# Squaring the clipped ramp on VectorE instead of ScalarE in a two-layer feed-forward kernel

## The chip, the cores and the metric

The kernel runs on one NeuronCore of a Trainium2 chip. The metric is device time in microseconds of one launch; the shorter the better. Weights, queries, keys and values start in device memory and the result ends there.

## What is computed

The reference is a windowed attention with attention sinks, and behind it two dense feed-forward layers of 1536 tokens, model width 512 and hidden width 2048, all in float32. The change touches the nonlinear function of the first feed-forward layer alone:

```python
h = x @ w_in                       # 1536 x 512 times 512 x 2048
beta = 1.0
neg = h <= -beta
pos = h >= beta
g = np.where(pos, h, np.where(neg, 0.0, (h + beta) ** 2 / (4.0 * beta)))
return (g @ w_out)                 # back to 1536 x 512
```

So g is 0 below -1, h above 1, and the square of r = relu(h/2 + 1/2) between. The second layer has an exponential in that place. Attention comes first and its output is the x of the first layer.

## The kernel before

The tokens of the first layer are worked in six chunks of 256 (the code numbers them 0 to 5), those of the second in three chunks of 512. A chunk walks over 16 tiles t of 128 hidden units. TensorE (PE) computes, in this order for each t: `hidden` (12 matmuls into the PSUM bank `h_ps`, lines 495 to 510), `outward` of tile t-2 (12 matmuls into `y_ps`, lines 512 to 527), and then the pieces of attention for the next chunk that the plan `BESIDE` puts on this t: values, transposes, scores. Every weight and activation is split in a high and a low float32r part, and each product takes three matmuls; ScalarE (ACT) casts the high part and VectorE (DVE) subtracts it to get the low one.

A tile of the first layer goes through these steps. ACT computes `ramp` from `h_ps` (line 670) and squares it in place (line 672); DVE takes min and max against h to make `g_full` (line 866, one instruction); ACT casts `g_hi` (`part_hi`, line 662) and DVE subtracts `g_lo` (`part_lo`, line 855). `hidden` of tile t+2 waits until `g_full` of tile t is there (its PSUM bank is then free), and `outward` of tile t waits for `g_lo`. `ramp` and `g_full` each have two buffers.

Each engine runs its own list in order, written out by hand. For one tile DVE's list is: `before_layer` (the split of the next head's keys and queries, lines 784 and 785, and the normalising of the softmax, lines 805 to 811), `part_lo` of the tile before, `activate`, `behind_layer` (row maxima, lines 797 and 800; the split of the sinks, lines 817 and 820) and, in chunk 0 on tiles 0 to 12 and in chunk 5 on even tiles, `split_weights` (line 842; one or two calls). ACT's list runs likewise: split of the head (593, 594), exponentials (603), `part_hi` (662), `activate` (670, 672), copy of the transposed probabilities (608 to 614), `write_x` (619), and the cast half of `split_weights` (644). DVE's line 842 waits for ACT's line 644, and ACT's line 603 waits for DVE's line 800. Heads are worked two per three tiles: scores at tiles 2, 3, 5, 6, 8, 9, 11, 12. GpSimd (POOL) issues the loads of keys, queries and values, and SyncE (SP) those of the weights and the stores. Chunks 0 to 4 carry attention for the chunk behind them; chunk 5 carries none, but splits weights of the second layer.

The constant 0.5 that line 670 uses as its bias lies in a tile `half` of 64 columns, and the row statistics in a tile `small` of 16 columns. Tiles made by `sb0` are for the first layer and are laid out behind `small`; the second layer's tiles reuse their place.

Of the kernel before, what the change touches and what calls it, by code (L numbers as in the profile page):

```python
# [26 lines left out]
ALU = mybir.AluOpType  # L27
ACT = mybir.ActivationFunctionType

P = 128  # L30
# [8 lines left out]
QB = CT // P  # L39
PAIRS = HEADS // 2  # L40
KT = DM // P
FT = DFF // P
# [36 lines left out]
IN_FLIGHT = 2  # L79


def build(nc, qk_first, v_first, q_t, k_t, v_w, v_s, w_in, w_out, ident_d, out, n_sink, window):
# [8 lines left out]
    with ExitStack() as ctx:  # L91
        def sb(name, shape, dt=F32):
            return ctx.enter_context(nc.sbuf_tensor(name, shape, dt))

        def ps(name):
            return ctx.enter_context(nc.psum_tensor(name, [P, 512], F32))

        def sem(name):
            return ctx.enter_context(nc.semaphore(name))
# [5 lines left out]
        xy = sb("xy", [P, KT, TOK])  # L105
        ident = sb("ident", [P, P])

        small = sb("small", [P, IN_FLIGHT * 4 * QB])
        tops, totals = (small[:, n:n + IN_FLIGHT * 2 * QB].rearrange("p (s h j) -> p s h j", s=IN_FLIGHT, h=2)
                        for n in (0, IN_FLIGHT * 2 * QB))  # L110
        top, total = tops[:, 0, :, :], totals[:, 0, :, :]

        first_layer = ctx.enter_context(ExitStack())

        def sb0(name, shape, dt=F32):
            return first_layer.enter_context(nc.sbuf_tensor(name, shape, dt))
# [1 line left out]
        x_hi, x_lo = sb0("x_hi", [P, KT, CT], F32R), sb0("x_lo", [P, KT, CT], F32R)  # L118
        g_hi, g_lo = sb0("g_hi", [P, GR, CT], F32R), sb0("g_lo", [P, GR, CT], F32R)
        ramp, g_full = sb0("ramp", [P, 2, CT]), sb0("g_full", [P, 2, CT])  # L120
        half = sb0("half", [P, 64])


        qs, ks = sb0("qs", [P, 2, CT]), sb0("ks", [P, 2, QB * SW])
# [21 lines left out]
        t_ps, o_ps = ps("t_ps"), ps("o_ps")  # L146
# [16 lines left out]
        ramp_ready, g_hi_ready, x_hi_ready, y_written, w_hi_ready = sem("ramp_ready"), sem("g_hi_ready"), sem("x_hi_ready"), sem("y_written"), sem("w_hi_ready")  # L163
        bent_ready, qk_hi_ready, qk_lo_ready = sem("bent_ready"), sem("qk_hi_ready"), sem("qk_lo_ready")
# [3 lines left out]
        g_ready, g_lo_ready, x_lo_ready, w_lo_ready = sem("g_ready"), sem("g_lo_ready"), sem("x_lo_ready"), sem("w_lo_ready")  # L168
# [8 lines left out]
        def layer_tiles(layer):  # L177

            if layer == 0:
                return CT, (x_hi, x_lo), (g_hi, g_lo), ramp, g_full  # L180
            return CT1, (x1_hi, x1_lo), (g1_hi, g1_lo), ramp1, g1_full
# [236 lines left out]
        def _(pe):  # L418
# [21 lines left out]
            def first_values(p):  # L440
                pe.wait_ge(first_v_loaded[p], 16)
                pe.wait_ge(first_copied, 2 * (p + 1))
                if p >= IN_FLIGHT:
                    pe.wait_ge(x_lo_ready, p - IN_FLIGHT + 1)
                _, o_bank, _, probs_t = flight[p % IN_FLIGHT]

                for block, queries, keys_t in ((0, slice(0, CT), slice(0, CT)), (1, slice(P, CT), slice(CT, CT + P))):
                    for hh in range(2):
                        dims = slice(HD * hh, HD * (hh + 1))
                        last = pe.matmul(o_bank[dims, queries], first_v[p][:, block * P + HD * hh:block * P + HD * (hh + 1)],  # L450
                                         probs_t[hh][:, keys_t], start=(block == 0), stop=(block == 1), skip_group_check=True)
                last.then_inc(first_attn, 1)
# [42 lines left out]
            def hidden(layer, c, t):  # L495

                pe.wait_ge(w_hi_ready, at[layer * NW + 2 * (t // 2)] + 1)
                pe.wait_ge(w_lo_ready, at[layer * NW + 2 * (t // 2)] + 1)
                if t >= 2:
                    pe.wait_ge(g_ready, c * FT + (t - 1))  # L500
                width, (x_hi, x_lo), _, _, _ = layer_tiles(layer)
                o = h_ps[t % 2][:, 0:width]
                f = slice(t * P, (t + 1) * P)
                for k in range(KT):
                    if t == 0:
                        pe.wait_ge(x_lo_ready, c * KT + (k + 1))
                    pe.matmul(o, win_hi[:, k, f], x_hi[:, k, :], start=(k == 0), stop=False)  # L507
                    pe.matmul(o, win_hi[:, k, f], x_lo[:, k, :], start=False, stop=False)  # L508
                    last = pe.matmul(o, win_lo[:, k, f], x_hi[:, k, :], start=False, stop=(k == KT - 1))  # L509
                last.then_inc(h_ready, 1)  # L510

            def outward(layer, c, t):


                pe.wait_ge(w_lo_ready, at[layer * NW + 2 * (t // 2) + 1] + 1)
                pe.wait_ge(g_lo_ready, c * FT + (t + 1))
                _, _, (g_hi, g_lo), _, _ = layer_tiles(layer)
                for m in range(KT):
                    o = y_of(layer, m)
                    begin = t == 0 and (layer == 1 or m % 2 == 0)  # L520
                    cols = slice(m * P, (m + 1) * P)
                    pe.matmul(o, wout_hi[:, t, cols], g_hi[:, t % GR, :], start=begin, stop=False, skip_group_check=True)  # L522
                    pe.matmul(o, wout_hi[:, t, cols], g_lo[:, t % GR, :], start=False, stop=False, skip_group_check=True)  # L523
                    last = pe.matmul(o, wout_lo[:, t, cols], g_hi[:, t % GR, :], start=False, stop=(t == FT - 1), skip_group_check=True)  # L524
                    if layer == 1 and t == FT - 1 and m < KT - 1:
                        last.then_inc(y_done, 1)
                last.then_inc(y_step, 1)
# [36 lines left out]
        def _(act):  # L564
            def first_exponents(p):
                banks = flight[p % IN_FLIGHT][0]
                act.wait_ge(first_neg_max, p + 1)
                if p >= IN_FLIGHT:
                    act.wait_ge(first_probs_t, 2 * (p - IN_FLIGHT + 1))
                for hh in range(2):  # L570
                    for j in range(QB):
                        nc.scalar.activation(seen_probs(p, hh)[:, SEEN_OF[j]], banks[hh][:, SEEN_OF[j]], ACT.Exp,
                                             bias=tops[:, p % IN_FLIGHT, hh, j:j + 1],
                                             accum_out=totals[:, p % IN_FLIGHT, hh, j:j + 1]).then_inc(first_exp, 1)
# [89 lines left out]
            def activate(layer, c, t):  # L664
                act.wait_ge(h_ready, c * FT + (t + 1))
                width, _, _, ramp, g_full = layer_tiles(layer)
                h = h_ps[t % 2][:, 0:width]
                if layer == 0:

                    nc.scalar.activation(ramp[:, t % 2, :], h, ACT.Relu, bias=half[:, 0:1], scale=0.5).then_inc(ramp_ready, 1)  # L670
                    act.wait_ge(ramp_ready, c * FT + (t + 1))
                    nc.scalar.activation(ramp[:, t % 2, :], ramp[:, t % 2, :], ACT.Square).then_inc(bent_ready, 1)  # L672
                else:

                    nc.scalar.activation(ramp[:, 0, :], h, ACT.Relu, scale=-1.0).then_inc(ramp_ready, 1)  # L675
                    act.wait_ge(ramp_ready, c * FT + (t + 1))
                    nc.scalar.activation(g_full[:, t % 2, :], ramp[:, 0, :], ACT.Exp, scale=-1.0).then_inc(bent_ready, 1)  # L677
# [39 lines left out]
            act.wait_ge(half_set, 1)  # L717
            act.wait_ge(zeros_set, 1)

            nc.scalar.activation(t_ps[:, 0:1], half[:, 0:1], ACT.Exp)  # L720
            first_exponents(0)
            first_exponents(1)
            for p in range(PAIRS):
# [23 lines left out]
        def _(dve):  # L747
# [110 lines left out]
            def activate(layer, c, t):  # L858
                width, _, _, ramp, g_full = layer_tiles(layer)
                h = h_ps[t % 2][:, 0:width]  # L860
                g = g_full[:, t % 2, :]
                if layer == 0:


                    dve.wait_ge(bent_ready, c * FT + (t + 1))
                    nc.vector.scalar_tensor_tensor(g, h, 1.0, ramp[:, t % 2, :], ALU.max, ALU.min).then_inc(g_ready, 1)  # L866
                else:

                    dve.wait_ge(bent_ready, c * FT + (t + 1))
                    nc.vector.scalar_tensor_tensor(g, g, -1.0, h, ALU.add, ALU.max).then_inc(g_ready, 1)  # L870
# [110 lines left out]
```

## Time and profile before

| | us |
|---|---|
| three runs | 642.58, 643.86, 646.44 (median 643.86) |
| the profiled execution | 642.58 |
| its span, first to last instruction | 640.9 |
| PE busy | 620.9 (97% of the span) |
| ACT busy | 388.2 (61%) |
| DVE busy | 339.5 (53%) |
| POOL busy | 74.7 (12%) |

The time of the profiled execution is 1.7 us longer than its span. Busy shares are means over stages that differ much: in the first 80 us DVE and ACT are busy nearly all the time, in the second layer (from about 374 us on) less than half of it. TensorE's granted clock was 0.999 of full speed over the whole span. Matmuls overlap one another, so a PE that is "busy" all the time can still have small holes.

### The profile page before, as it was taken

To read this page: it belongs to the slowest core of one execution; us is meant where nothing else is said; L and a number is where in the kernel's file an instruction comes from. 1 tells how busy PE (TensorE), PEld (TensorE's weight loads), DVE (VectorE), ACT (ScalarE), POOL (GpSimd) and SP (SyncE) were. 2 spreads that over 40 slices of the span, in tenths; PEclk is the share of its full clock that TensorE was granted. 3 is DMA by queue.
4 is the path that set the end of the run, shared out by engine and by line. 5 is a ranking of instruction groups with operands and counts; after the bars stand their busy time and mean duration, and the time that the engine had idled before them with its cause. 6 is when DMAs were issued, how large, how long until landed. Compare 5 with 4: busy or idle time off the path is not lost.

```text
span 640.9 us, 12200 instructions
## 1 busy us (share of the span) xinstructions
PE 620.9 (97%) x4164; PEld 554.8 (87%) x4164; DVE 339.5 (53%) x898; ACT 388.2 (61%) x926; POOL 74.7 (12%) x147
## 2 busy tenths in 40 slices
PE   5799999999999999999999999999999999999997
PEld 3688899999999999999999988888888888888886
DVE  6799948666775677477646663322332222322221
ACT  5888867876876787777767764333443333533333
POOL 5213203221221223123000000000000000000000
PEclk9999999999999999999999999999999999999999
DMA  7764212321321222123045600000100000100001
GB/s 272 236 220 144 68 39 73 98 66 31 98 89 39 64 89 89 33 70 103 0 166 164 197 1 0 1 1 1 66 0 0 0 1 1 65 0 0 0 0 65
DMA packets 15276, 42.49 MB, mean 66 GB/s; under 512 B 2852, under 2 KB 4536, under 8 KB 15248
## 3 DMA queue, kind: packets, MB, share of 16 engines
q0 software_dynamic: 7040, 20.57, 10.6%
q1 hardware_dynamic: 8208, 21.56, 9.8%
q8 instruction: 15, 0.25, 0.2%
q14 instruction: 13, 0.11, 0.1%
HBM read 38.98 MB, written 3.15 MB: 66 GB/s over the span
## 4 chain that ended last, share of the span: by engine, by line
PE 85%; DVE 7%; ACT 5%; issue 2%; DMA 0%; ACTq 0%; SPq 0%; DVEq 0%
PE h_ps L507 13%; PE h_ps L509 13%; PE h_ps L508 12%; PE y_ps L522 9%; PE y_ps L524 9%; PE y_ps L523 9%; PE s_ps L524 3%; PE s_ps L523 3%; PE s_ps L522 3%; PE o_ps L490 3%; PE t_ps L470 2%; DVE wout_lo L842 1%; PE s_ps L461 1%; PE s_ps L460 1%; DVE win_lo L842 1%
## 5 line engine op out<-in xcount | busy, mean ns | idle before, releaser
L507 PE MATMUL h_ps<-x_hi,win_hi 128*128 128x256 f32 (+1 forms) x576 | 184.7, 321 | 0.6 <-DVE g_full L866 0.3
L509 PE MATMUL h_ps<-x_hi,win_lo 128*128 128x256 f32 (+1 forms) x576 | 182.8, 317 | 0.0
L508 PE MATMUL h_ps<-x_lo,win_hi 128*128 128x256 f32 (+1 forms) x576 | 182.4, 317 | 0.0
L522 PE MATMUL y_ps<-g_hi,wout_hi 128*128 128x256 f32 (+1 forms) x480 | 145.5, 303 | 1.8 <-DVE g_lo L855 1.8
L524 PE MATMUL y_ps<-g_hi,wout_lo 128*128 128x256 f32 (+1 forms) x480 | 144.9, 302 | 0.0
L523 PE MATMUL y_ps<-g_lo,wout_hi 128*128 128x256 f32 (+1 forms) x480 | 144.8, 302 | 0.0
L507 PEld LDWEIGHTS h_ps<-x_hi,win_hi 128*128 128x128 f32 x576 | 108.1, 188 | 10.1 <-DVE g_full L866 1.1
L508 PEld LDWEIGHTS h_ps<-x_lo,win_hi 128*128 128x128 f32 x576 | 108.1, 188 | 8.4
L509 PEld LDWEIGHTS h_ps<-x_hi,win_lo 128*128 128x128 f32 x576 | 108.2, 188 | 7.2
L870 DVE SCALAR_TENSOR_TENSOR g_full<-g_full,h_ps 128x512 f32<-128x512 f32 x48 | 33.0, 688 | 151.9 <-ACT g_full L677 151.9
L855 DVE TENSOR_TENSOR g_lo<-g_full,g_hi 128x256 fp32r<-128x256 f32 (+1 forms) x144 | 73.7, 512 | 53.3 <-ACT g_hi L662 52.6
L675 ACT ACTIVATE ramp<-h_ps 128x512 f32<-128x512 f32 x48 | 28.8, 599 | 117.4 <-PE h_ps L509 116.8
L662 ACT CAST g_hi<-g_full 128x256 fp32r<-128x256 f32 (+1 forms) x144 | 68.4, 475 | 49.9 <-DVE g_full L870 34.1
L522 PEld LDWEIGHTS y_ps<-g_hi,wout_hi 128*128 128x128 f32 x480 | 90.1, 188 | 7.3 <-DVE g_lo L855 1.4
L523 PEld LDWEIGHTS y_ps<-g_lo,wout_hi 128*128 128x128 f32 x480 | 90.0, 187 | 4.2
L524 PEld LDWEIGHTS y_ps<-g_hi,wout_lo 128*128 128x128 f32 x480 | 90.2, 188 | 3.6
L866 DVE SCALAR_TENSOR_TENSOR g_full<-h_ps,ramp 128x256 f32<-128x256 f32 x96 | 40.2, 419 | 22.1 <-ACT ramp L672 22.0
L670 ACT ACTIVATE ramp<-h_ps,half 128x256 f32<-128x256 f32 x96 | 45.5, 474 | 6.0 <-PE h_ps L509 5.8
L603 ACT ACTIVATE probs<-s_ps,small 128x260 f32<-128x260 f32 x80 | 37.3, 471 | 19.1 <-DVE small L800 19.0
L377 POOL DMA_DIRECT2D ks<-in_k x40 | 22.1, 553 | 209.6 <-DVE q_parts L785 208.0
L672 ACT ACTIVATE ramp<-ramp 128x256 f32<-128x256 f32 x96 | 40.1, 418 | 3.0
L524 PE MATMUL s_ps<-g_hi,wout_lo 128*128 128x512 f32 x96 | 37.8, 394 | 0.0
(109 smaller groups left out, 814.0 us busy)
## 6 DMA issues: line engine op xcount, KB each, us to landing
ks<-in_k POOLq DMA_DIRECT2D x40, 260.0 KB, 2.9
raw<-in_w_in SPq DMA_DIRECT2D x11, 512.0 KB, 4.3
raw<-in_w_out SPq DMA_DIRECT2D x11, 512.0 KB, 3.9
qs<-in_q POOLq DMA_DIRECT2D x40, 128.0 KB, 2.7
vals<-in_v POOLq DMA_DIRECT2D x20, 192.0 KB, 3.0
out_y<-xy SPq DMA_DIRECT2D x12, 256.0 KB, 2.1
xy<-in_w_in SPq DMA_DIRECT2D x5, 512.0 KB, 5.1
xy<-in_w_out SPq DMA_DIRECT2D x5, 512.0 KB, 4.1
```

What stands on the lines that cost most here:

```text
L507: pe.matmul(o, win_hi[:, k, f], x_hi[:, k, :], start=(k == 0), stop=False)
L508: pe.matmul(o, win_hi[:, k, f], x_lo[:, k, :], start=False, stop=False)
L509: last = pe.matmul(o, win_lo[:, k, f], x_hi[:, k, :], start=False, stop=(k == KT - 1))
L522: pe.matmul(o, wout_hi[:, t, cols], g_hi[:, t % GR, :], start=begin, stop=False, skip_group_check=True)
L523: pe.matmul(o, wout_hi[:, t, cols], g_lo[:, t % GR, :], start=False, stop=False, skip_group_check=True)
L524: last = pe.matmul(o, wout_lo[:, t, cols], g_hi[:, t % GR, :], start=False, stop=(t == FT - 1), skip_group_check=True)
L603: nc.scalar.activation(probs[:, j, hh * SW:(hh + 1) * SW], s_ps[j][:, 0:SW], ACT.Exp, bias=top[:, hh, j:j + 1], accum_out=total[:, hh, j:j ...
L662: nc.scalar.copy(g_hi[:, t % GR, :], g_full[:, t % 2, :]).then_inc(g_hi_ready, 1)
L670: nc.scalar.activation(ramp[:, t % 2, :], h, ACT.Relu, bias=half[:, 0:1], scale=0.5).then_inc(ramp_ready, 1)
L672: nc.scalar.activation(ramp[:, t % 2, :], ramp[:, t % 2, :], ACT.Square).then_inc(bent_ready, 1)
L855: nc.vector.tensor_tensor(g_lo[:, t % GR, :], g_full[:, t % 2, :], g_hi[:, t % GR, :].bitcast(F32), ALU.subtract).then_inc(g_lo_ready, 1)
L866: nc.vector.scalar_tensor_tensor(g, h, 1.0, ramp[:, t % 2, :], ALU.max, ALU.min).then_inc(g_ready, 1)
```

## The change

The square of the ramp is no longer computed by ACT but by DVE, as min(r, 1) * r into `g_full`; the last step is then a plain maximum with h. Both forms give the same function: where r is over 1, r is at most h, so the maximum with h gives h. DVE now waits for `ramp_ready` in place of `bent_ready`, and waits for its own first instruction before the second reads its result. The constant 0.5 moves from its own tile of 64 columns into one column of `small`, which grows from 16 to 32 columns, and the first-layer tiles behind move accordingly: those in front of the old place of `half` 64 bytes up, those behind it 192 bytes down.

```diff
-        small = sb("small", [P, IN_FLIGHT * 4 * QB])
+        small = sb("small", [P, 2 * IN_FLIGHT * 4 * QB])
+        half = small[:, IN_FLIGHT * 4 * QB:IN_FLIGHT * 4 * QB + 1]
-        half = sb0("half", [P, 64])
...
                 if layer == 0:
                     nc.scalar.activation(ramp[:, t % 2, :], h, ACT.Relu, bias=half[:, 0:1], scale=0.5).then_inc(ramp_ready, 1)
-                    act.wait_ge(ramp_ready, c * FT + (t + 1))
-                    nc.scalar.activation(ramp[:, t % 2, :], ramp[:, t % 2, :], ACT.Square).then_inc(bent_ready, 1)
...
-            nc.scalar.activation(t_ps[:, 0:1], half[:, 0:1], ACT.Exp)
+            nc.scalar.activation(t_ps[:, 0:1], half[:, :], ACT.Exp)
...
                 if layer == 0:
+                    r = ramp[:, t % 2, :]
+                    dve.wait_ge(ramp_ready, c * FT + (t + 1))
+                    nc.vector.scalar_tensor_tensor(g, r, 1.0, r, ALU.min, ALU.mult).then_inc(bent_ready, 1)
                     dve.wait_ge(bent_ready, c * FT + (t + 1))
-                    nc.vector.scalar_tensor_tensor(g, h, 1.0, ramp[:, t % 2, :], ALU.max, ALU.min).then_inc(g_ready, 1)
+                    nc.vector.tensor_tensor(g, g, h, ALU.max).then_inc(g_ready, 1)
```

## Rows read from the trace of the kernel before

**Rows 1.** The page's first line: the span, and how many instructions.

```profile
span 640.9 us, 12200 instructions
```

**Rows 2.** The chain that ended last: start us, length us, engine, tile, line.

```profile
25.35 0.48 ACT ramp L670
...
91.12 0.48 ACT ramp L670
...
150.68 0.48 ACT ramp L670
151.18 0.43 ACT ramp L672
151.64 0.44 DVE g_full L866
```

**Rows 3.** Busy us (and count) of each engine in two stretches, then clock and DMA.

```profile
64.00:80.00 16.00, 14.95 (x125) 13.85 (x124) 14.71 (x39) 14.38 (x38) 4.69 (x7) 1.00 0.23 69
160.00:192.00 32.00, 32.00 (x279) 30.96 (x278) 24.01 (x81) 25.70 (x75) 8.21 (x16) 1.00 0.31 94
```

**Rows 4.** Line 866 among the groups: count, busy us, mean ns, idle before it.

```profile
L866 DVE SCALAR_TENSOR_TENSOR g_full<-h_ps,ramp 128x256 f32<-128x256 f32 x96 | 40.2, 419 | 22.1 <-ACT ramp L672 22.0
```

**Rows 5.** Timeline of DVE in chunk 0: start, length, instruction, idle before it.

```profile
26.31 0.42 DVE L866 SCALAR_TENSOR_TENSOR g_full<-h_ps,ramp 128x256 f32<-128x256 f32 x1 [0.19 <-ACT ramp L672]
27.25 1.23 DVE L842 TENSOR_TENSOR wout_lo<-xy,wout_hi 128x1024 fp32r<-128x1024 f32 x1 [0.51 <-ACT wout_hi L644]
...
29.31 1.23 DVE L842 TENSOR_TENSOR win_lo<-xy,win_hi 128x1024 fp32r<-128x1024 f32 x1 [0.17 <-ACT win_hi L644]
...
40.41 1.22 DVE L842 TENSOR_TENSOR wout_lo<-xy,wout_hi 128x1024 fp32r<-128x1024 f32 x1 [0.60 <-ACT wout_hi L644]
...
60.64 0.42 DVE L785 TENSOR_TENSOR q_parts<-qs,q_parts 64x256 fp32r<-64x256 f32 x1
61.09 0.17 DVE L805 TENSOR_SCALAR small<-small 128x2 f32<-128x2 f32 x1
...
62.37 0.41 DVE L866 SCALAR_TENSOR_TENSOR g_full<-h_ps,ramp 128x256 f32<-128x256 f32 x1
62.70 0.42 DVE L797 CUSTOM_DVE_ANT_0 s_ps<-s_ps,mask 128x260 f32<-128x260 f32 x1
...
67.41 1.23 DVE L842 TENSOR_TENSOR wout_lo<-xy,wout_hi 128x1024 fp32r<-128x1024 f32 x1 [0.85 <-ACT wout_hi L644]
```

**Rows 6.** Timeline of ACT in chunk 0, around tile 10.

```profile
65.02 0.49 ACT L670 ACTIVATE ramp<-h_ps,half 128x256 f32<-128x256 f32 x1
...
65.86 0.57 ACT L608 COPY probs_t<-t_ps 128x512 f32<-128x512 f32 x1
66.33 1.05 ACT L644 CAST wout_hi<-xy 128x1024 fp32r<-128x1024 f32 x1
```

**Rows 7.** Timeline of PE: the first matmul of outward(12) in chunk 0.

```profile
80.24 0.36 PE L522 MATMUL y_ps<-g_hi,wout_hi 128*128 128x256 f32 x1 [0.20 <-DVE g_lo L855]
```

**Rows 8.** Timeline of DVE in chunk 2: its idle times within three tiles.

```profile
161.59 0.17 DVE L805 TENSOR_SCALAR small<-small 128x2 f32<-128x2 f32 x1 [0.77 <-ACT probs L603]
...
163.71 0.70 DVE L784 TENSOR_TENSOR k_lo<-ks,k_hi 128x520 fp32r<-128x520 f32 x1 [0.76 <-ACT q_parts L594]
...
166.06 0.44 DVE L797 CUSTOM_DVE_ANT_0 s_ps<-s_ps,mask 128x260 f32<-128x260 f32 x1 [0.42 <-PE s_ps L461]
```

**Rows 9.** Timeline of PE in chunk 2: the first matmul of hidden(6).

```profile
165.94 0.28 PE L507 MATMUL h_ps<-x_hi,win_hi 128*128 128x256 f32 x1
```

**Rows 10.** Timelines of DVE and PE at the end of chunk 5.

```profile
367.93 1.23 DVE L842 TENSOR_TENSOR win_lo<-raw,win_hi 128x1024 fp32r<-128x1024 f32 x1 [0.52 <-ACT win_hi L644]
...
371.43 0.43 DVE L855 TENSOR_TENSOR g_lo<-g_full,g_hi 128x256 fp32r<-128x256 f32 x1 [0.47 <-ACT g_hi L662]
...
370.77 0.36 PE L522 MATMUL y_ps<-g_hi,wout_hi 128*128 128x256 f32 x1 [0.54 <-DVE g_lo L855]
...
372.26 0.28 PE L522 MATMUL y_ps<-g_hi,wout_hi 128*128 128x256 f32 x1
```

## The prediction

> **What bounds the kernel now.** I read the chain that ended last first, then the busy times by stretch, then the timelines of DVE, ACT and PE where the chain leaves PE. The span is 640.9 us [rows 1]. The first ramp of each chunk is on that chain [rows 2]: chunk 0 at 25.35, chunk 1 at 91.12, chunk 2 at 150.68. So chunk 1 takes 59.56 us and chunk 0 takes 65.77, 6.2 us more for the same matmuls. The stretches say why [rows 3]: from 160 to 192 us PE is busy for 32.00 of 32 us, DVE for 24.01 and ACT for 25.70; from 64 to 80 us PE has holes (14.95 of 16), and DVE (14.71) and ACT (14.38) are nearly full, since chunk 0 also splits weights. The kernel is bound by PE, except in chunk 0, where DVE and ACT in turn set the pace up to tile 12, and at single points. The change takes a square from ACT for each of the 96 tiles [rows 4] and gives DVE an instruction more. Its effect must come mainly from chunk 0, where 13 of them lie before the point at which PE takes over for good.
>
> **What one tile costs DVE and gives ACT.** DVE keeps one instruction of the old size (the maximum, with one PSUM input; line 866 takes 419 ns [rows 4]) and gets one more in front of it, whose two inputs are the same SBUF tile. Where nothing holds the next instruction, DVE starts it before the last has ended: 62.37 to 62.70, 0.33 us for a length of 0.41, an overlap of 0.08 [rows 5]. Where the next has to come after the last is complete, the overlap is lost: 60.64 to 61.09, 0.45 us for a length of 0.42 [rows 5]. The new instruction has 256 columns too and its follower waits for its completion, so I take 0.42 + 0.03 = **0.45 us per tile**. Below it the nearest rows are 0.33 (a free follower) and 0.17 + 0.03 = 0.20 (line 805, with hardly any columns). Above it I see nothing dearer for 256 columns except an instruction that pays its length and gap twice, 0.90. I keep 0.20 and 0.90 as ends and sit on 0.45, from the row nearest in size and kind of follower.
>
> The Trainium skill, "VectorE: DVE Perf Modes", section "The DRAIN you can't avoid", says that a semaphore between two VectorE instructions costs nothing extra, since the next waits for the pipe to empty anyway. The rows don't bear that out: 0.33 against 0.45. By that rule the price is the free one, 0.33, and the sum below is +0.7 us instead of +2.0; it is within the third rival.
>
> ACT loses the square. From the ramp to the copy behind the square it now takes 65.02 to 65.86, 0.84 us; without the square it is the ramp's 0.49 less the 0.10 by which a free follower overlaps on ACT (65.86 to 66.33 for a length of 0.57), so 0.39 [rows 6]. ACT gains **0.45 per tile**; bounds: 0.33 and 0.53, the square's length of 0.43 [rows 2] less and plus the overlap.
>
> The way of one tile through both engines keeps its length: ramp at 150.68, square at 151.18, line 866 from 151.64 to 152.08 [rows 2]; new: the ramp ends at 151.16, then 0.03 to the other engine, 0.42, 0.03, 0.42: 152.06. Where PE waits for g_full of tile 0 at a chunk's start, nothing changes.
>
> **Chunk 0, step by step.** The chain here is a loop of three tiles (two heads). DVE splits weights (line 842) and works through two tiles up to the row maxima (line 800); ACT takes over with exponentials, part_hi, ramp, square, a copy and the weight cast, and DVE's next line 842 waits for that cast. The DVE piece holds two of the new instructions, the ACT piece one square. A new line 842 starts at the later of two: ACT's cast, 0.45 earlier against the lag so far, or DVE's own list, 0.45 later less its slack. The slack is the idle time before line 842 plus the overlap of 0.08 that a free follower would have: 0.51 + 0.08 and 0.17 + 0.08 in tiles 0 and 1, 0.60 + 0.08 in tile 4, 0.85 + 0.08 in tile 10 [rows 5] and, alike, in tile 7. As lags against the old times:
> - tile 0: line 866 was 0.19 late for want of the square [rows 5]; 0.45 - 0.19 - 0.59 = -0.33.
> - tile 1: DVE -0.33 + 0.45 - 0.25 = **-0.13**; ACT, 0.45 earlier twice, comes before that.
> - tiles 2 and 3 +0.90; tile 4: DVE +0.77 + 0.45 - 0.68 = **+0.54**, ACT +0.77 - 0.45 = +0.32.
> - tiles 5 and 6 +0.90; tile 7: DVE 1.44 + 0.45 - 0.93 = +0.96, ACT **+0.99**.
> - tiles 8 and 9 +0.90; tile 10: DVE 1.89 - 0.48 = +1.41, ACT **+1.44**.
> - tiles 11 and 12 +0.90: **+2.34**. Then DVE makes g_lo of tile 12, for which PE waits until 80.24 [rows 7].
>
> From there PE works through its list, so the 2.3 us stay. 13 x 0.45 would be 5.9; DVE's idle time takes up more than half. At tile 7 and 10 the two engines come out even: neither has anything left to give.
>
> **Chunks 1 to 4.** DVE's idle times in three tiles are 0.77, 0.76 and 0.42 [rows 8], 1.95 us, and it gets 1.35. Followed through: the maxima of tile 3 come 0.45 later, so do the exponentials and, in front of tile 4, line 805 at 161.59. Tile 4 adds 0.45; ACT, without its square, begins copy and head split on time, so line 784 is 0.90 - (0.76 + 0.08) = 0.06 late. Tile 5 adds 0.45 and line 797 is 0.51 - (0.42 + 0.08) = 0.01 late, where it waits for PE's scores. So the lag is gone once per loop. The latest result in between is g_full of tile 4, 0.90 late; it stands directly before line 784 in DVE's list, so it is there by 163.85, and PE takes it for hidden of tile 6 at 165.94 [rows 9]. Cost 0; what it costs if this cover goes is a rival below.
>
> **Chunk 5 and the rest.** PE waits 0.54 us at 370.77 for g_lo of tile 14 [rows 10]. On DVE that stands behind two weight splits, the first of which (367.93) waits 0.52 for ACT's cast, and the cast stands behind a square. The cast comes 0.45 earlier. DVE must be ready as early: its slack there is 0.52 + 0.08 = 0.60, and where line 866 itself waited for the square, as it does for 22.0 us in sum over the kernel [rows 4], the pair in its place ends no later than it did. So g_lo of tile 14 comes 0.45 earlier. Tile 15 then waits for its own way through both engines, which is no shorter: its g_lo ends at 371.86 and PE starts some 0.1 later, at about 371.96 against 372.26 [rows 10]. PE gains 0.3. The second layer is PE's alone and its instructions are the same. Setting one column in place of 64 lies in the first microsecond, before the loads have landed. The shift of tiles by 64 or 192 bytes I take as 0: no row shows any effect of a tile's place, and the only bound either way is the spread of the three runs, 3.9 us.
>
> **Sum.** 2.3 - 0.3 = +2.0 us: the profiled execution goes from 642.58 to 644.6, its span from 640.9 to 642.9. That execution was the fastest of three and the median lies 1.28 higher, so I predict 645.9.
>
> **Rivals.**
> - *Nothing is absorbed.* If DVE's idle before line 842 isn't filled, because ACT's cast comes no earlier (the copy before it waiting for PE's transposes), each of 13 tiles costs 0.45: 5.85 - 0.3 = +5.6, 649.5. For it: both engines wait for each other in a loop. Against: the copy at 65.86 followed the square at once [rows 6], with nothing else awaited.
> - *Chunks 1 to 4 become DVE's.* With the three overlaps DVE's slack in a loop is 0.85 + 0.84 + 0.50 = 2.19 us [rows 8], so it is the bound from 2.19 / 3 = 0.73 us per tile on. At 0.90, the upper end, each loop loses 3 x 0.17 = 0.51; with 4 loops (8 heads) in each of 4 chunks that is 8 us, and chunk 0 gets 13 x 0.45 = 5.9 more than in the walk: +16, about 660. Against: no instruction of 256 columns costs that.
> - *The new instruction is cheap.* At 0.33 the same walk gives +1.0 in chunk 0, at 0.20 it gives -0.3; in all +0.7 or -0.6, 643.3 to 644.6.
> - *ACT's relief wins.* Five pieces of the chain in chunk 0 hold a square (tiles 0, 1, 4, 7, 10), one in chunk 5. If ACT decides at all of them, it takes off 5 x 0.45 = 2.25, against eight DVE instructions on the chain (tiles 2, 3, 5, 6, 8, 9, 11, 12): faster from a price below 2.25 / 8 = 0.28 on; at a price of 0 it would be -2.6, 641.3. Against: 0.20 is the least that any row shows, and there it is worth half a microsecond.
>
> **How the numbers follow.** The walk as worked out 0.58, nothing absorbed 0.17, chunks 1 to 4 0.07, a cheap instruction 0.12, ACT's relief 0.06. About 0.5% (3.2 us) is what a measurement of this kernel can tell from no change. Slower by more: the second and third case and 0.05 of the first by the spread of runs, 0.29. Faster by more: 0.05 of the last, with the shift of tiles. The rest, 0.66, is within. The range goes from 643.0 (a cheap instruction and a little spread) to 650.0 (nothing absorbed, and half a microsecond).
>
> **What would show it.** Right if in the profile after the first ramps of chunk 0 and 1 are about 68.1 us apart and the later ones still 59.5; if the new instruction is 0.42 us long and 0.45 ahead of the maximum; if DVE's idle before line 842 in chunk 0 is nearly gone; if DVE's busy time is up and ACT's down by 40 us each; if PE's wait at the end of chunk 5 splits into about 0.1 at tile 14 and 0.2 at tile 15. Wrong if chunks 1 to 4 grow, if the pair is spaced otherwise, or if idle time stays before line 842.

## The result and the profile after

| | before | after |
|---|---|---|
| median of six runs, us | 643.87 (642.58 to 646.44) | 651.98 (650.91 to 654.3) |
| ratio, 95% interval | | 1.0127 (1.0104 to 1.0149) |
| profiled execution, us | 642.58 | 650.88 |
| its span, us | 640.9 | 649.1 |

The change made the kernel slower by 1.3%, 8.1 us. The forecast was 645.9 with a range of 643.0 to 650.0; the time lies outside it, and every rival but one (660, for chunks 1 to 4) ended below it too.

The page of after, its span, busy times and chain by engine:

```profile
span 649.1 us, 12200 instructions
...
PE 628.1 (97%) x4164; PEld 558.4 (86%) x4164; DVE 377.9 (58%) x994; ACT 349.4 (54%) x830; POOL 74.7 (12%) x147
```

DVE is busy 38.4 us more and ACT 38.8 us less, as the change intends. But PE is busy 7.2 us more, with the same 4164 instructions. That is the first sign that something acts on PE itself, and not through a wait.

Next I took the first ramps of the chunks, as in [rows 2]. The timeline of ACT in after (start, length, instruction, idle time before it):

```profile
25.23 0.47 ACT L670 ACTIVATE ramp<-h_ps,small 128x256 f32<-128x256 f32 x1 [0.42 <-PE h_ps L509]
...
93.44 0.47 ACT L670 ACTIVATE ramp<-h_ps,small 128x256 f32<-128x256 f32 x1 [0.19 <-PE h_ps L509]
...
153.36 0.47 ACT L670 ACTIVATE ramp<-h_ps,small 128x256 f32<-128x256 f32 x1 [0.19 <-PE h_ps L509]
...
380.89 0.60 ACT L673 ACTIVATE ramp<-h_ps 128x512 f32<-128x512 f32 x1 [1.63 <-PE h_ps L509]
```

From such rows of both traces comes the table on which everything below rests, in us:

| stretch | before | after | difference |
|---|---|---|---|
| start to the first ramp | 25.35 | 25.23 | -0.12 |
| chunk 0 | 65.77 | 68.21 | +2.44 |
| chunks 1 to 4 | 59.56, 59.45, 59.55, 59.21 | 59.92, 59.97, 59.94, 59.75 | +1.81 |
| chunk 5 | 47.74 | 47.87 | +0.13 |
| second layer, from its first ramp on | 264.27 | 268.21 | +3.94 |

Chunk 0 is where the walk put its 2.3 us. Nearly all of the rest, 5.75 us, lies in stretches for which the prediction had 0, and the largest piece lies in the second layer, where no instruction was changed. The first 512-token chunk of that layer, stretch by stretch (start and end, length, then busy us and count of PE, PEld, DVE, ACT, POOL, then clock, DMA share, GB/s), first before:

```profile
376.63:464.52 87.89, 87.89 (x385) 72.12 (x384) 27.94 (x39) 36.57 (x59) 0.00 (x0) 1.00 0.03 13
```

and after:

```profile
380.89:470.13 89.24, 89.24 (x385) 72.35 (x384) 27.96 (x39) 36.48 (x60) 0.00 (x0) 1.00 0.03 12
```

PE is busy all the time in both, the granted clock is 1.00 in both, DVE, ACT and DMA do the same work. So the 384 matmuls have become dearer. The timeline of PE in before, four matmuls in a row:

```profile
400.46 0.39 PE L522 MATMUL s_ps<-g_hi,wout_hi 128*128 128x512 f32 x1
400.69 0.39 PE L523 MATMUL s_ps<-g_lo,wout_hi 128*128 128x512 f32 x1
400.92 0.39 PE L524 MATMUL s_ps<-g_hi,wout_lo 128*128 128x512 f32 x1
401.15 0.39 PE L507 MATMUL h_ps<-x_hi,win_hi 128*128 128x512 f32 x1
```

and the same four in after:

```profile
405.09 0.39 PE L522 MATMUL s_ps<-g_hi,wout_hi 128*128 128x512 f32 x1
405.32 0.40 PE L523 MATMUL s_ps<-g_lo,wout_hi 128*128 128x512 f32 x1
405.55 0.40 PE L524 MATMUL s_ps<-g_hi,wout_lo 128*128 128x512 f32 x1
405.79 0.40 PE L507 MATMUL h_ps<-x_hi,win_hi 128*128 128x512 f32 x1
```

Three starts take 0.69 us before and 0.70 after. A difference of 1.5% can't be read from rows with two decimals; it can from a stretch: 87.89 / 384 = 0.2289 us from start to start before, 89.24 / 384 = 0.2324 after. In the code of this layer nothing differs but where its tiles lie. Hence the theory for the experiments: *place*, the time of a matmul depends on the address of what it reads. Its rival: *computation*, the new instruction on DVE costs more than the walk says, beside PE's work too.

Medians of the same kernel differ by some 2 us from one set of runs to another (before: 643.2, 645.1, 643.8, 644.0), because some of its executions spend 2 to 4 us more in front of the first ramp (27.5 to 29.0 us in such profiles instead of 25.2 to 26.2), so ratios are taken within a set, and lengths of chunks, which this doesn't touch, are compared across all profiles and are the finer measure.

### The profile page after: what moved, and what is told of

Same layout as the page of the kernel before. It is cut to its first block, busy times and chain, and to the rows that moved or that the text cites. A ratio compares the mean times of both kernels' runs of the same rounds, so it can differ in the third digit from the quotient of the medians.

```text
span 649.1 us, 12200 instructions
## 1 busy us (share of the span) xinstructions
PE 628.1 (97%) x4164; PEld 558.4 (86%) x4164; DVE 377.9 (58%) x994; ACT 349.4 (54%) x830; POOL 74.7 (12%) x147
## 4 chain that ended last, share of the span: by engine, by line
PE 86%; DVE 9%; ACT 2%; issue 1%; DMA 0%; ACTq 0%; SPq 0%; DVEq 0%
PE h_ps L507 13%; PE h_ps L509 13%; PE h_ps L508 13%; PE y_ps L522 10%; PE y_ps L523 9%; PE y_ps L524 9%; PE s_ps L522 3%; PE s_ps L523 3%; PE s_ps L524 3%; PE o_ps L490 3%; PE t_ps L470 2%; DVE wout_lo L840 1%; PE s_ps L461 1%; PE s_ps L460 1%; DVE win_lo L840 1%
## 5 line engine op out<-in xcount | busy, mean ns | idle before, releaser
L507 PE MATMUL h_ps<-x_hi,win_hi 128*128 128x256 f32 (+1 forms) x576 | 186.7, 324 | 0.8 <-DVE g_full L866 0.4
L522 PE MATMUL y_ps<-g_hi,wout_hi 128*128 128x256 f32 (+1 forms) x480 | 147.0, 306 | 1.8 <-DVE g_lo L853 1.8
L670 ACT ACTIVATE ramp<-h_ps,small 128x256 f32<-128x256 f32 x96 | 45.5, 474 | 6.0 <-PE h_ps L509 6.0
L864 DVE SCALAR_TENSOR_TENSOR g_full<-ramp 128x256 f32<-128x256 f32 x96 | 40.3, 420 | 9.4 <-ACT ramp L670 9.2
L866 DVE TENSOR_TENSOR g_full<-g_full,h_ps 128x256 f32<-128x256 f32 x96 | 40.4, 421 | 3.3
```

The lines of the kernel that those rows point to most:

```text
L864: nc.vector.scalar_tensor_tensor(g, r, 1.0, r, ALU.min, ALU.mult).then_inc(bent_ready, 1)
L866: nc.vector.tensor_tensor(g, g, h, ALU.max).then_inc(g_ready, 1)
```

## The experiments

For orientation in what follows: the weights (`win_hi`, `win_lo`, `wout_hi`, `wout_lo`) lie in front of `small`, and what a matmul streams past them (`x_hi`, `x_lo`, `g_hi`, `g_lo` and the second layer's `x1_hi`, `g1_hi` and so on) lies behind it. The change moves all of the latter by 64 or -192 bytes, which is the same step of 64 within 256 (that 256 is the period is shown by e5 and e8 below).

**Splitting the change (e1, e2).** e1 is the kernel before with the change's layout alone:

```diff
-        small = sb("small", [P, IN_FLIGHT * 4 * QB])
+        small = sb("small", [P, 2 * IN_FLIGHT * 4 * QB])
+        half = small[:, IN_FLIGHT * 4 * QB:IN_FLIGHT * 4 * QB + 1]
-        half = sb0("half", [P, 64])
```

> The kernel before with only the tiles moved: small has 32 columns, half is one of them, ACT still squares. The measured change is +8.2 us of span, of which chunk 0 shows +2.4 (as the walk of the prediction gave), chunks 1 to 4 about +0.4 each and each chunk of the second layer +1.3, though no instruction differs there. Theory P (the place of the tiles in SBUF slows PE's matmuls, pitch 0.2289 to 0.2324 us in the second layer): this kernel loses about 5.9 us, 649.8, with 16-tile chunks of the second layer at 89.2 us and chunk 0 unchanged at 65.8. Theory D (the work moved to DVE costs it, also later): this kernel is as before, 643.9, second-layer chunks 87.9 us. Theory R (the difference of the second layer is chance of that profiled execution): also 87.9.

e2 is the other half: the square on DVE, with `small` and `half` as before.

```diff
-                    act.wait_ge(ramp_ready, c * FT + (t + 1))
-                    nc.scalar.activation(ramp[:, t % 2, :], ramp[:, t % 2, :], ACT.Square).then_inc(bent_ready, 1)
...
+                    nc.vector.scalar_tensor_tensor(g, r, 1.0, r, ALU.min, ALU.mult).then_inc(bent_ready, 1)
```

> The kernel after with the tiles where they were before: small 16 columns, half a tile of 64 columns; DVE squares and ACT does not. Theory P: +2.0 us against before, 645.9, the number of the prediction: chunk 0 at 68.2 us, chunks 1 to 4 at 59.5, second-layer chunks 87.9. Theory D: +8, 652.0, and second-layer chunks 89.2.

Measured: e1 651.87 us, ratio 1.0113 (1.0085 to 1.0141); e2 645.57 us, 1.0028 (1.0011 to 1.0044). The second layer's first chunk of e1, stretch as above:

```profile
381.89:471.13 89.24, 89.24 (x385) 72.34 (x384) 27.96 (x39) 36.59 (x59) 0.00 (x0) 1.00 0.03 12
```

and of e2 chunk 0, chunk 1 and the same chunk of the second layer:

```profile
25.25:93.34 68.09, 61.74 (x510) 57.28 (x509) 62.04 (x163) 49.85 (x123) 13.46 (x23) 1.00 0.40 126
93.34:152.90 59.56, 59.23 (x510) 56.85 (x509) 47.08 (x148) 38.46 (x111) 13.67 (x25) 1.00 0.23 71
...
377.58:465.47 87.89, 87.89 (x385) 72.11 (x384) 27.95 (x39) 36.51 (x59) 0.00 (x0) 1.00 0.03 11
```

e1 has after's second-layer chunk to the hundredth (89.24) with before's computation, and chunks 1 to 4 of 59.96, 59.98, 59.95, 59.70. Its ratio says 7.3 us, more than the 5.9 expected; its chunks add up to 6.3. e2 has before's (87.89), chunks of 59.56, 59.56, 59.55, 59.33, and a chunk 0 of 68.09. So the two halves of the change act apart: the layout costs 1.8 us in chunks 1 to 4 and 4.0 in the second layer; the computation costs 2.3 in chunk 0. Its rival, that the computation costs more beside PE's work, falls: 0.2 us in chunks 1 to 4 together. e2 has one oddity: its chunk 5 takes 46.24 instead of 47.74, though no tile was moved, and that is why its profiled span is only 0.9 us above before's. That execution is also the shortest of e2's twelve (643.52 against a median of 645.57), so not every execution need have it.

The oddity is not e2's alone: at this distance matmuls of 256 columns keep one of two pitches, 0.1133 or 0.1178 us, and both occur in before. In chunk 2 of before there are 22 steps from 152.34 to 154.83, 0.113 us each, and 22 from 185.82 to 188.41, 0.118 each (timeline of PE, first and last row of each stretch):

```profile
152.34 0.28 PE L508 MATMUL h_ps<-x_lo,win_hi 128*128 128x256 f32 x1
154.83 0.28 PE L524 MATMUL y_ps<-g_hi,wout_lo 128*128 128x256 f32 x1
...
185.82 0.28 PE L508 MATMUL h_ps<-x_lo,win_hi 128*128 128x256 f32 x1
188.41 0.28 PE L524 MATMUL y_ps<-g_hi,wout_lo 128*128 128x256 f32 x1
```

Nearly all the rest of before's chunks 1 to 5 runs at the longer pitch; one more such stretch lies in chunk 4. e2's chunk 5 runs at the shorter one in one piece of 334 steps, from behind the chunk's first tile up to PE's wait at tile 14, and the ten steps behind the wait at tile 15 are back at 0.118. So the pitch is kept while nothing interrupts the stream and can change where something does. What chooses between the two isn't shown.

**Absolute place or distance (e3, e4).** e3 puts a spare tile of 128 bytes behind `small`, so only what is streamed moves; e4 puts one of 64 bytes in front of the weights, so all moves together.

```diff
+        spare = sb("spare", [P, 32])      # e3: behind small
...
+        spare0 = sb("spare0", [P, 16])    # e4: in front of win_hi
```

> The kernel before with a spare tile of 32 columns (128 bytes) behind small, so that all tiles behind it lie 128 bytes up. If what matters is the place of the matmuls' moving tiles within 128 bytes (now 64 past a multiple of 128, after the change on a multiple), this kernel is as fast as before, 643.9, pitch 0.229. If any move away from the old place costs, or the period is longer, it is slower, up to 650.

> The kernel before with a spare tile of 16 columns (64 bytes) in front of the weights, so that weights and all other tiles lie 64 bytes up together. If it is the absolute place of the moving tiles that matters, this kernel is slow like the changed one, near 650 with a pitch of 0.232. If it is their place relative to the weights, it is as before, 643.9 with 0.229.

Measured: e3 643.92, ratio 1.0000 (0.9978 to 1.0022); e4 643.72, 0.9998 (0.9977 to 1.0018). e4 is before again in every chunk (59.56, 59.45, 59.54, 59.22; 87.89). e3's equal total hides two effects of opposite sign, as its chunk 1 and the second layer show:

```profile
94.18:152.65 58.47, 58.16 (x510) 55.81 (x509) 40.69 (x132) 44.65 (x127) 13.66 (x25) 1.00 0.25 72
...
374.24:463.84 89.60, 89.60 (x385) 72.19 (x384) 27.96 (x39) 36.59 (x59) 0.00 (x0) 1.00 0.03 12
```

The attention chunks are 1.1 us shorter each, the second layer's 1.7 longer. It isn't the address of a tile that counts but the distance from the weights to it, and the two widths of matmul (256 and 512 columns) like different distances. For 256 columns the step from before's distance to e3's brings no new pitch but more of the shorter one: e3's chunk 1 has 0.1178 in its tiles 1 to 3 and 0.1135 to 0.114 from tile 4 on, where before has 0.1178 in all of these.

**Mapping the distance (e5, e7, e8, e9).** Here the first layer's tiles and the second layer's move separately, by a spare tile in front of `x_hi` (n columns) and one in front of `g1_hi` (m columns); the second layer's reuse the place of the first, so their shift doesn't include n. e5: n 32, m 128; e7: 48, 48; e8: 64, 64; e9: 32, 48.

```diff
+        spare = sb0("spare", [P, n])
         x_hi, x_lo = sb0("x_hi", [P, KT, CT], F32R), sb0("x_lo", [P, KT, CT], F32R)
...
+        spare1 = sb("spare1", [P, m])
```

> The kernel before with its first-layer tiles 128 bytes up (a spare tile of 32 columns) and its second-layer tiles 512 bytes up (a spare tile of 128 columns), weights untouched. With everything 128 up the chunks with attention took 58.46 us in place of 59.5 and those of the second layer 89.6 in place of 87.9. Theory P (only the distance of moving tile and weights counts, layer by layer, and it repeats with the weights' own step of 512 bytes): 4 x 1.1 + 1.4 less in the first layer, the second unchanged at 87.9, so about 5.7 us less than before: 637.5, faster than both kernels. If it does not repeat after 512 bytes, the second layer stays at 89 or more and the whole at 643. If the two layers' times were tied in some other way (clock, chance), nothing like 637 comes.

> The kernel before with the tiles of both layers 192 bytes up, 256 past the weights' step where it was 64. If a distance that is a multiple of 128 is bad (as 128 was), chunks with attention 59.95 us and second-layer chunks 89.2 or more: 650. If the times fall and rise with a period of 128 bytes only, they are those of 128. If the distance acts over the whole 512 bytes, other numbers than the three known.

> The kernel before with the tiles of both layers 256 bytes up, distance 320. With a period of 256 bytes it is as before: 59.5 and 87.9 us per chunk, 643.2. With a period of 128 bytes likewise. With one of 512, other numbers: it then says which way the second layer goes beyond 192, where it had 89.6.

> The computation of the kernel before, with each layer's tiles where its matmuls were fastest so far: first-layer tiles 128 bytes up (58.4 us per chunk with attention), second-layer tiles 192 bytes up (87.04 us per chunk). Theory P: 4 x 1.1 + 1.3 + 3 x 0.86 = 8.3 us less than before, 635 us. If the two gains don't add, no better than 639.

Measured: e5 639.07, ratio 0.9909 (0.9880 to 0.9939); e7 645.98, 1.0011 (0.9990 to 1.0032); e8 643.51, 0.9989 (0.9968 to 1.0009); e9 636.61, 0.9884 (0.9853 to 0.9915). Chunk 1 and the second layer's first chunk of e7:

```profile
93.97:154.13 60.16, 59.92 (x510) 57.54 (x509) 40.82 (x132) 44.83 (x127) 13.62 (x25) 1.00 0.24 70
...
382.79:469.83 87.04, 87.04 (x385) 72.07 (x384) 27.90 (x39) 36.56 (x59) 0.00 (x0) 1.00 0.03 12
```

and the second layer's first chunk of e9:

```profile
373.14:460.18 87.04, 87.04 (x385) 72.07 (x384) 27.91 (x39) 36.56 (x59) 0.00 (x0) 1.00 0.03 12
```

Shifts of 256 (e8) and 512 bytes (e5's second layer, 87.90) give before's chunks back. With the distance of before counted as 64, chunks 1 to 3 and the second layer of all these profiles fit one table (chunk 5 doesn't, as e2 shows):

| distance, bytes within 256 | attention chunk, us | second-layer chunk, us (per matmul) | seen in |
|---|---|---|---|
| 64 | 59.5 | 87.9 (0.2289) | before, e2, e4, e8, e10, e11; e5 (second layer) |
| 128 | 59.95 | 89.24 (0.2324) | after, e1 |
| 192 | 58.4 | 89.60 (0.2333) | e3; e5, e9, e12, e14 (first layer) |
| 0 | 60.16 | 87.04 (0.2267) | e7; e9, e12, e14 (second layer) |

The change took the kernel from the first row to the second, the second worst for either layer. e9 takes the best row for each layer and is 1.2% faster than before, with before's computation untouched.

**Which tiles make the pair (e6, e13).** e6 moves the second layer's `x1_hi`, `x1_lo` and `raw1` by 64 bytes and leaves `g1_hi` and `g1_lo`. e13 moves the weights `win_hi` and `win_lo` away from everything behind them, by a spare tile between them and `wout_hi`.

```diff
+        spare1 = sb("spare1", [P, 16])    # e6: in front of x1_hi, behind g1_hi and g1_lo
...
+        spare = sb("spare", [P, 16])      # e13: between win_lo and wout_hi
```

> The kernel before with only x1_hi, x1_lo and raw1 64 bytes up (a spare tile of 16 columns in front of x1_hi), as the change does with all tiles; g1_hi and g1_lo stay. If a matmul's pitch follows the place of its own moving tile, the hidden product (lines 507 to 509) slows from 0.2289 to 0.2324 us as in the changed kernel and the outward product (522 to 524) keeps its pitch: 87.9 + 0.67 = 88.6 us per chunk, 2.0 us in all, 645.3. If PE is slowed by traffic of the other engines at that place, both products slow or neither does.

> The kernel before with a spare tile of 64 bytes between win_lo and wout_hi, so that win_hi and win_lo stay, and wout_hi, wout_lo and every tile behind (raw, xy, ident, small, the tiles of both layers) lie 64 bytes up. The moving tiles of the hidden product are then 64 bytes farther from their weights, those of the outward product as far as before, and all moving tiles as far from xy, raw and small as before. Theory P (distance to the matmul's own weights): second-layer pitch 0.232 to 0.235 on lines 507 to 509, about 0.230 on 522 to 524 as with x1 alone, 88.8 us per chunk, 646. If it is the distance to tiles other than the weights that counts, 87.9 us per chunk, 643.5. If it is the absolute place, 89.2 us.

Measured: e6 645.88, ratio 1.0023 (1.0005 to 1.0040), first layer as before, second-layer chunks 88.80 and 88.82; e13 647.04, 1.0059 (1.0030 to 1.0089), chunks 59.73, 59.74, 59.75, 59.51 and 88.66, 88.74. Both lie between 87.9 and 89.24. Where they differ from before is seen from the first matmul of a product to the first of the next, 12 matmuls on. In e13 (line 508 is `hidden`, line 523 `outward`) `hidden` takes 2.79 us and `outward` 2.75:

```profile
402.89 0.39 PE L508 MATMUL h_ps<-x_hi,win_hi 128*128 128x512 f32 x1
...
405.68 0.39 PE L523 MATMUL y_ps<-g_hi,wout_hi 128*128 128x512 f32 x1
...
408.43 0.39 PE L508 MATMUL h_ps<-x_hi,win_hi 128*128 128x512 f32 x1
```

and in before, where they are lines 507 and 522, 2.75 and 2.74:

```profile
401.15 0.39 PE L507 MATMUL h_ps<-x_hi,win_hi 128*128 128x512 f32 x1
...
403.90 0.39 PE L522 MATMUL y_ps<-g_hi,wout_hi 128*128 128x512 f32 x1
...
406.64 0.39 PE L507 MATMUL h_ps<-x_hi,win_hi 128*128 128x512 f32 x1
```

The mean of all such starts in the second layer, in us per matmul:

| | hidden | outward |
|---|---|---|
| before | 0.2289 | 0.2289 |
| after | 0.2324 | 0.2323 |
| e6, x1 moved | 0.2328 | 0.2298 |
| e13, win moved | 0.2325 | 0.2295 |

The single pitches within a product are no guide: in before they go round 0.2258, 0.2292 and 0.2317, and in e4, which has before's mean, the same three stand one matmul further on. In e6 and e13 alike `hidden`, whose streamed tile and weights are now 128 apart, has about after's mean, and `outward`, whose pair is where it was, is near before's. So what counts is a matmul's moving tile against the weights of its own product, not against other tiles. What `outward` has above 0.2289 sits at its ends: in e13 in its last matmul (0.2349; those in the middle have 0.2289), in e6 in its first two (0.2333 and 0.2348). In the trace the weights of the next matmul are loaded while one streams, so these means would be nearly the same if it were the next matmul's weights that count; the two aren't told apart.

**The computation alone (e10, e11).** The walk says that the square on DVE costs in eight tiles of chunk 0 and gains in five, and once in chunk 5. Both kernels keep before's layout and put the square on DVE only for a list of tiles; for these ACT leaves it out.

```diff
+ON_DVE = [(0, 0), (0, 1), (0, 4), (0, 7), (0, 10), (5, 14)]    # e10
+ON_DVE = [(0, 2), (0, 3), (0, 5), (0, 6), (0, 8), (0, 9), (0, 11), (0, 12)]    # e11
...
+                    if on_dve(c, t):
...
+                        nc.vector.scalar_tensor_tensor(g, r, 1.0, r, ALU.min, ALU.mult).then_inc(bent_dve, 1)
+                        dve.wait_ge(bent_dve, ON_DVE.index((c, t)) + 1)
+                        nc.vector.tensor_tensor(g, g, h, ALU.max).then_inc(g_ready, 1)
```

> All tiles where they were before. The square is on DVE only for tiles 0, 1, 4, 7 and 10 of chunk 0 and tile 14 of chunk 5, the ones after which DVE waits for ACT's weight cast. By the walk of the prediction (0.45 each way): tile 1 -0.13, tile 4 -0.36, tile 7 -0.81, tile 10 -1.26, so chunk 0 takes 64.5 us in place of 65.8, and PE's wait at the end of chunk 5 shrinks by 0.3: 641.6 against 643.2. If DVE is simply the bound of chunk 0, five more instructions there cost 5 x 0.45: 68.0 us for chunk 0.

> All tiles where they were before. The square is on DVE only for tiles 2, 3, 5, 6, 8, 9, 11 and 12 of chunk 0, where the chain runs through DVE. By the walk nothing absorbs them: 8 x 0.45 = +3.6, chunk 0 takes 69.4 us. At the free pitch of 0.33 it would be +2.6, 68.4. If what counts is DVE's total of work, 8 of 13 instructions cost 8/13 of the +2.3 measured: 67.2.

Measured: e10 642.93, ratio 0.9973 (0.9952 to 0.9995); e11 646.32, 1.0042 (1.0019 to 1.0065). The timeline of ACT in e10, first ramps of chunk 0 and 1:

```profile
27.50 0.47 ACT L676 ACTIVATE ramp<-h_ps,half 128x256 f32<-128x256 f32 x1 [1.38 <-PE h_ps L515]
...
91.93 0.48 ACT L676 ACTIVATE ramp<-h_ps,half 128x256 f32<-128x256 f32 x1
```

and in e11:

```profile
25.35 0.48 ACT L676 ACTIVATE ramp<-h_ps,half 128x256 f32<-128x256 f32 x1 [0.41 <-PE h_ps L515]
...
94.52 0.48 ACT L676 ACTIVATE ramp<-h_ps,half 128x256 f32<-128x256 f32 x1
```

Chunk 0 takes 64.43 in e10 (-1.34) and 69.17 in e11 (+3.40; 0.425 for each of eight tiles); chunk 5 takes 47.28 in e10 (-0.46). And the idle time of 0.85 us that DVE had before the weight split of tile 10 [rows 5] is still there in e11, where no tile relieves ACT:

```profile
70.09 1.23 DVE L851 TENSOR_TENSOR wout_lo<-xy,wout_hi 128x1024 fp32r<-128x1024 f32 x1 [0.85 <-ACT wout_hi L650]
```

So the loop of three tiles is as the walk had it: on the chain two DVE instructions and one ACT square per turn.

**Together (e12, e14).** e12 is e10's computation in e9's layout; e14 is the change's whole computation in e9's layout.

```diff
+ON_DVE = [(0, 0), (0, 1), (0, 4), (0, 7), (0, 10), (5, 14)]    # e12; in e14 all tiles, as in the change
...
+        spare = sb0("spare", [P, 32])
...
+        spare1 = sb("spare1", [P, 48])
```

> The two together: squares on DVE in the six relief tiles, tiles placed as in the fastest layout. -8.3 and -1.6: 633.3 us, faster than before by 1.5%. If a faster PE leaves less room for the relief in chunk 0 it is the same there, since chunk 0 is set by DVE and ACT: then 64.5 us for chunk 0 all the same.

> The changed computation (DVE squares every tile of the first layer) in the fastest layout, first-layer tiles 128 and second-layer tiles 192 bytes up. Against the same layout with the computation of before (636.6 measured): chunk 0 +2.3 as before (68.1), chunk 5 -0.3 (its fast pitch is already there, so not the -1.5 seen with the tiles in the old place), chunks 1 to 4 unchanged at 58.4: 638.5. If the computation costs more on a faster PE, because chunks 1 to 4 come near DVE's bound, they take over 58.6 us.

Measured: e12 633.00, ratio 0.9842 (0.9814 to 0.9869); e14 638.97, 0.9916 (0.9887 to 0.9946). The page of e12:

```profile
span 631.1 us, 12206 instructions
```

Chunk 1 of e14:

```profile
96.84:155.26 58.42, 58.09 (x510) 55.75 (x509) 46.70 (x148) 38.06 (x110) 13.61 (x25) 1.00 0.24 72
```

e12 beats both kernels: its span is 1.5% below before's (631.1 against 640.9) and 2.8% below after's (649.1), and its median 1.6% below before's. e14 has e9's short chunks although DVE does every square; only its chunk 2 is longer, 58.71 against 58.46. It takes 2.4 us more than e9's 636.61 (across sets of runs), 2.2 by the chunks, and again the loss is in chunk 0: 67.91 against 65.79. What the change's computation costs by the sum of the chunks is 2.1 us in the change's own layout (after against e1), 2.2 in e9's, and 1.0 in before's, where e2's profile has the short chunk 5; e2's median says 1.8.

## Why the prediction was wrong, step by step

**The failed step: "The shift of tiles by 64 or 192 bytes I take as 0."** e1 measures it alone: +1.13%, 7.3 us by the ratio; by the chunks, +1.8 in chunks 1 to 4 and +4.0 in the second layer, with 0.2 in chunk 0 and 0.3 in chunk 5, 6.3 us. Of the 8.2 us between the two spans this is three quarters. The reason given, that no row shows an effect of a tile's place, was true and no evidence: in a single trace every tile has one place. The bound put beside it, 3.9 us from the spread of the runs, was no bound on this effect either. With PE busy for 620.9 us, 1% on every matmul would be 6 us: an estimate, not a measurement, but it shows how much the 0 staked. The other terms held (2.1 us measured between e1 and after, 2.0 forecast), so the miss is this term's alone.

**The pitch and the read ports.** The mean pitch of the matmuls in the second layer's chunks goes from 0.2267 (e7) to 0.2333 us (e3) by the distance alone. The Trainium skill, "TensorE: Matmul & The Clock Gate", section "Step-by-step: what each phase is for", says that PE has two independent read ports, so that loading the next weights takes no read bandwidth from the running matmul. Whoever reads that as "where the two lie doesn't matter" gets 0 for the shift; for these float32r matmuls the measured pitches say otherwise. That it is the weight load that disturbs isn't shown.

**The price of the pair, 0.45 us per tile: right.** The timeline of DVE in after, at tile 10 of chunk 0:

```profile
67.54 0.42 DVE L853 TENSOR_TENSOR g_lo<-g_full,g_hi 128x256 fp32r<-128x256 f32 x1
67.88 0.42 DVE L864 SCALAR_TENSOR_TENSOR g_full<-ramp 128x256 f32<-128x256 f32 x1
68.33 0.42 DVE L866 TENSOR_TENSOR g_full<-g_full,h_ps 128x256 f32<-128x256 f32 x1
68.70 1.23 DVE L840 TENSOR_TENSOR wout_lo<-xy,wout_hi 128x1024 fp32r<-128x1024 f32 x1
```

and ACT's cast for its last row:

```profile
67.59 1.07 ACT L644 CAST wout_hi<-xy 128x1024 fp32r<-128x1024 f32 x1
```

The new instruction starts at 67.88, the maximum that waits for it at 68.33, 0.45 us on, and so it is in all 96 tiles (0.45 to 0.46). The free follower in front comes after 0.34; the split behind comes after 0.37, but it waits for ACT's cast, which ends at 68.66. So the waited step costs 0.1 us more than the free one, and e11's 0.425 per tile, on the chain, agrees better with 0.45 than with 0.33. That the value came out is in part luck: the row it was read from isn't of the kind the prediction took it for. Line 805, at 61.09 [rows 5], doesn't wait for line 785 but for ACT's exponentials, the last of which ends at 59.98; it starts only behind the end of line 785 all the same, and why isn't shown. ACT's gain was right too: from the ramp to the copy it takes 0.37 in after (66.76 to 67.13) where it took 0.84. And at chunk 2's start the way from ramp to `g_full` is 1.39 us in after and 1.40 in before, unchanged as said. The rule of the Trainium skill weighed in the prediction ("VectorE: DVE Perf Modes", "The DRAIN you can't avoid": the semaphore costs nothing) isn't borne out here. The split at 68.70 answers to the last of [rows 5]: 1.29 us later, or 1.41 counted from the chunk's first ramp, which is 0.12 earlier in after (said: tile 10 at +1.44), and no longer with idle time before it.

**The walk through chunk 0: right.** Said +2.34; measured +2.44 in after and +2.32 in e2. Line 842 of before (840 in after) starts at tile 0 at 26.82 and at tile 1 at 29.08; from the chunk's first ramp that is -0.31 and -0.11 against before (said -0.33 and -0.13). Tile 4 is at +0.58 (said +0.54) and tile 7 at +0.98 (said +0.99).

```profile
26.82 1.22 DVE L840 TENSOR_TENSOR wout_lo<-xy,wout_hi 128x1024 fp32r<-128x1024 f32 x1
...
29.08 1.22 DVE L840 TENSOR_TENSOR win_lo<-xy,win_hi 128x1024 fp32r<-128x1024 f32 x1
```

PE's wait at tile 12 [rows 7] ends 2.16 us later, 2.28 from the first ramp:

```profile
82.40 0.36 PE L522 MATMUL y_ps<-g_hi,wout_hi 128*128 128x256 f32 x1 [0.64 <-DVE g_lo L853]
```

**Chunks 1 to 4 at 0: right for the computation** (e2: 0.00, 0.11, 0.00, 0.12; the 0.1 in chunks 2 and 4 is what before saves by its 22 steps at the shorter pitch, which e2 has at the longer one, so nothing is left for DVE). DVE's idle time before line 805 of before [rows 8] is kept at 0.77, and the two behind it are filled, as said. The test named beforehand, "wrong if chunks 1 to 4 grow", came out against the forecast; the chunks grew by place, not by DVE, and it took e1 and e2 to tell the two apart.

**Chunk 5 at -0.3: right in kind.** In after PE's one wait of 0.54 us [rows 10] has become two of some 0.2, at tiles 14 and 15 (said 0.1 and 0.2). Against e1, in the same layout, that is -0.17; place takes it back, so after is 0.13 above before. Where only tile 14's square is moved (e10) it is -0.46, without the second wait.

**The groups, as said:** the new instruction is 420 ns long, 96 times, and the wait for the square is now one for the ramp, 9.2 us in sum where it was 22.0 [rows 4]. Both instructions take 0.42 us:

```profile
L866 DVE TENSOR_TENSOR g_full<-g_full,h_ps 128x256 f32<-128x256 f32 x96 | 40.4, 421 | 3.3
L864 DVE SCALAR_TENSOR_TENSOR g_full<-ramp 128x256 f32<-128x256 f32 x96 | 40.3, 420 | 9.4 <-ACT ramp L670 9.2
```

**The rivals.** Nothing absorbed (+5.6) comes nearer the total than the walk, but by accident; e2's chunk 0 (+2.3 and not +5.9) and the missing idle time refute it. "Chunks 1 to 4 become DVE's" is refuted by e2, the cheap instruction by the 0.45. ACT's relief is real, as e10 shows, and doesn't outweigh the eight other tiles.

## What to carry to other kernels

A change that resizes a small tile moves all tiles behind it, and that can cost or gain more than the change itself: compare first against the same kernel with the layout alone changed. In a kernel that PE fills, take a stretch with the same instructions in both and divide its length by the number of matmuls; if the pitch differs at the same clock, no wait explains it. And when two engines take turns on a chain, move work from one to the other tile by tile, only where the giver is late, not for all tiles.

## What the runs showed of the hardware that I had not expected

- In this kernel the mean pitch of float32r matmuls of 512 columns depends on the distance in bytes between what they stream and their weights, and repeats with 256 bytes: 0.2267, 0.2289, 0.2324 and 0.2333 us at distances 0, 64, 128 and 192 (as counted here), a spread of 2.9%. The attention chunks, where matmuls of 256 columns are the most of it, have another order: 58.4 at 192, 59.5, 59.95, and 60.16 at 0. Moving everything together by 64 bytes changes nothing (e4).
- At distances 64 and 192 matmuls of 256 columns keep one of two pitches, 0.1133 or 0.1178 us: both occur in before and in e3, and nearly all of e2's chunk 5 has the shorter one, though nothing was moved. Over that chunk it is 1.5 us.
- Why distance matters isn't shown. That the weight load and the matmul in flight disturb each other's reads would fit, and was only argued. Also open: what chooses between the two pitches, and whether the weights of the running or of the next matmul count.
- A VectorE instruction of 256 float32 columns that waits for the one before costs about 0.1 us more than one that doesn't (0.45 against 0.33 to 0.34), though a row of before has 0.45 without such a wait.
